# Attention and two expert layers on one core: heads of a pair on the two halves of the array, v as the stationary operand, tile loops written out

## The reference

```python
# attention: B=2, H=8, S=576, D=64
scores = scale * q @ k.T                      # scale = 1/8
kth = the 32nd largest score of each row
scores = where(scores >= kth, scores, -1e9)
attn = exp(scores - rowmax); attn /= attn.sum(-1) + 1e-9
x = attn @ v                                  # -> x: (1152, 512), token by (head, d)
# first layer: 1152 tokens, 512 -> 1536 -> 512
x = ((x @ w_a) * (x @ w_b)) @ w_out
# second layer: 4 experts, 512 -> 1024 -> 512
p = domain_probs / (domain_probs.sum(-1) + 1e-9)
out = sum over e of p[:, e] * (relu(x @ w1[e]) @ w2[e])
```

## Time and profile before

| | |
|---|---|
| median of 3 runs | 934.91 us (929.73, 935.0, 934.91) |
| the profiled execution | 931.27 us, span 929.5 us, so 1.8 us lie outside the span |
| PE busy (matmul) | 906.7 us, 98% of the span |
| DVE, ACT, POOL busy | 466.2, 356.3 and 386.4 us |
| mean granted PE clock | 0.969 of full speed |

### The profile page before, as it was taken

One profiled execution on the slowest core, in us unless ns is written; L12 is line 12 of the kernel. 1 busy time (PEld: TensorE's weight loads), 2 busy tenths in 40 slices (PEclk: granted clock), 3 DMA queues, 4 the chain that ended last, 5 costly groups with the idle time before them and its releaser, 6 DMA issues.

```text
span 929.5 us, 14737 instructions
## 1 busy us (share of the span) xinstructions
PE 906.7 (98%) x5012; PEld 803.7 (86%) x5012; DVE 466.2 (50%) x908; ACT 356.3 (38%) x748; POOL 386.4 (42%) x229
## 2 busy tenths in 40 slices
PE   6799999999999999999999999999999999999998
PEld 3567888888888888899999999889989988988997
DVE  4897899998888988962322222112112212221211
ACT  4465665655566656664332311023103301220110
POOL 2798877777666677672122130043003400070000
PEclk9575999999999999999999999999999999999999
DMA  7651000100000003313345020022000400000000
GB/s 200 134 137 41 16 24 23 30 26 24 24 24 26 24 23 115 115 39 104 102 148 216 1 90 2 0 89 92 0 0 8 173 0 0 0 0 23 11 34 34
DMA packets 63245, 50.40 MB, mean 54 GB/s; under 512 B 31840, under 2 KB 54368, under 8 KB 63200
## 3 DMA queue, kind: packets, MB, share of 16 engines
q1 hardware_dynamic: 58976, 43.55, 15.8%
q10 hardware_dynamic: 4224, 6.29, 2.1%
HBM read 40.39 MB, written 9.44 MB: 54 GB/s over the span
## 4 chain that ended last, share of the span: by engine, by line
PE 95%; SPq 2%; ACT 1%; DMA 1%; DVE 1%; issue 0%; ACTq 0%
PE ps L589 22%; PE ps L602 21%; PE ps L473 16%; PE ps L447 11%; PE ps L567 8%; PE ps L409 7%; PE ps L425 4%; PE ps L432 2%; PE ps L456 1%; SPq L265 1%; PE ps L406 1%; DMA v_sb<-v_in 1%; SPq L250 1%; PE ps L465 0%; SPq L256 0%
## 5 line engine op out<-in xcount | busy, mean ns | idle before, releaser
L985 POOL TENSOR_TENSOR w_lo<-w_raw,w_hi 128x2048 fp32r<-128x2048 f32 x16 | 74.1, 4654 | 307.8 <-ACT w_hi L695 307.8
L833 DVE MAX8 m<-work 128x8 f32<-128x576 f32 x216 | 152.3, 746 | 0.0
L770 ACT ACTIVATE h_hi<-ps 128x384 fp32r<-128x384 f32 x96 | 47.2, 492 | 272.5 <-PE ps L589 272.4
L944 POOL TENSOR_SCALAR p_sb<-s_sb,m 128x576 f32<-128x576 f32 x72 | 124.1, 1724 | 43.2 <-DVE m L833 43.2
L589 PE MATMUL ps<-x_hi,w_hi 128*128 128x384 f32 x384 | 128.5, 335 | 0.6 <-DVEq L906 0.6
L915 DVE SCALAR_TENSOR_TENSOR h_lo<-ps,h_hi 128x384 fp32r<-128x384 f32 x96 | 53.4, 557 | 150.1 <-ACT h_hi L770 150.0
L589 PE MATMUL ps<-x_lo,w_hi 128*128 128x384 f32 x384 | 128.4, 334 | 0.0
L589 PE MATMUL ps<-x_hi,w_lo 128*128 128x384 f32 x384 | 128.3, 334 | 0.0
L447 PEld LDWEIGHTS ps<-v_sb,pT 128*128 128x128 f32 (+3 forms) x800 | 101.0, 191 | 25.3 <-issue 15.3
L447 PE MATMUL ps<-v_sb,pT 128*128 128x65 f32 (+3 forms) x800 | 113.0, 282 | 2.1 <-ACT pT L651 2.1
L602 PE MATMUL ps<-w_lo,h_hi 128*128 128x512 f32 x288 | 113.5, 394 | 0.0
(11 more groups left out here) (87 smaller groups left out, 1589.5 us busy)
## 6 DMA issues: line engine op xcount, KB each, us to landing
w_raw<-moe_w_in SPq DMA_DIRECT2D x16, 1024.0 KB, 5.0
h<-hT SPq DMA_DIRECT2D x36, 192.0 KB, 2.1
h_raw<-h SPq DMA_DIRECT2D x9, 768.0 KB, 6.3
w_raw<-moe_w_a_in ACTq DMA_DIRECT2D x4, 768.0 KB, 6.3
w_raw<-moe_w_b_in ACTq DMA_DIRECT2D x4, 768.0 KB, 4.7
wo_raw<-moe_w_out_in SPq DMA_DIRECT2D x3, 1024.0 KB, 6.0
q_raw<-q_in SPq DMA_DIRECT2D x72, 32.0 KB, 2.2
v_sb<-v_in SPq DMA_DIRECT2D x18, 128.0 KB, 5.6
```

The source lines that it names most:

```text
L833: nc.vector.max(m8[:, par, i, 8 * r:8 * r + 8], work[:, i, :]).then_inc(ve_top, 1)
L944: nc.gpsimd.tensor_scalar(p_sb[:, ring, 0:S], s_sb[:, ring, :], m8[:, pr % 2, head, TOP_K - 1:TOP_K], None, ALU.is_ge).then_inc(po_m, 1)
L985: nc.gpsimd.tensor_tensor(lo[:, s, :], raw[s][:], hi[:, s, :].bitcast(F32), ALU.subtract).then_inc(done, 1)
```

## The change

Line numbers in the text are those of the kernel before, unless it says "after".

1. **Scores.** Both heads of a pair are done in one go, through four PSUM banks, head 0 and head 1 in turn, so that successive matmuls use rows 0 to 63 and rows 64 to 127 of the array. The four banks are shared with the transposes of p.
2. **Weighted sums.** v (128 keys by 64) is the stationary operand, the transposed p the moving one; the two heads write partitions 0 to 63 and 64 to 127 in turn. The result is x transposed, so the transpose of x falls away. The column of ones falls away too: the exponential of ACT gives the row sums (`accum_out`).
3. **Mask before exponential.** POOL adds -1e30 to the scores outside the 32 largest (`is_lt`, then `mult`, then an add), and ACT takes the exponential of that in place; before, the exponential came first and POOL multiplied it with the mask.
4. **Scaling.** The reciprocals are spread over the partitions by eight small matmuls with the identity (`inv_transpose`), copied by ACT (`inv_b`) and multiplied by POOL into x (`xu`); ACT makes the high part, POOL the low part.
5. **Order.** In a step of PE the h transpose stands ahead of both `up` products (before: between them), all transposes of p between them, and the weighted sums at the end. q of a whole tile is loaded and transposed at once; the first q is loaded by ACT's queue. On ACT both scores are copied together at the step's start.
6. **Loops.** All 44 steps are written out.

```diff
-            def scores(t, rep, pr, head):
...
-                pe.wait_ge(ac_s, n8)
-                rows = slice(head * D, (head + 1) * D)
-                for half in range(2):
...
-                        mm = nc.tensor.matmul(ps[:, half, 0:HALF], qT[rows, pr % 2, :], kT[rows, batch_of(rep), pr, cols],
-                                              start=True, stop=True)
+            def scores(n):
...
+                if n > LAG_PV:
+                    pe.wait_ge(ac_pT, 2 * (n - LAG_PV))
+                if n:
+                    pe.wait_ge(ac_s, 2 * n)
...
+                for half in range(2):
+                    cols = slice(half * HALF, (half + 1) * HALF)
+                    for tok, b in toks:
+                        for head in range(2):
+                            rows = slice(head * D, (head + 1) * D)
+                            mm = nc.tensor.matmul(ps[tok, 2 * head + half, 0:HALF], qT[rows, t % 2, pr, tok],
+                                                  kT[rows, b, pr, cols], start=True, stop=True)
+            def p_transpose(n):
+                for head in range(2):
+                    pe.wait_ge(ac_e, 2 * n + head + 1)
+                    pe.wait_ge(ac_s, 2 * min(n + LAG_PV, NP - 1) + head + 1)
...
+                for tok, b in toks:
+                    for c in range(KC):
+                        for head in range(2):
+                            mm = nc.tensor.matmul(ps_x[head * D:(head + 1) * D, pr * P + tok.start:pr * P + tok.stop],
+                                                  v_sb[b][:, c, 2 * pr + head, :], pT[:, head, c, tok],
+                                                  start=c == 0, stop=c == KC - 1)
+            def inv_transpose(t):
+                pe.wait_ge(ve_den, 2 * t + 2)
+                pe.wait_ge(ac_t, T_USE["inv", t])
+                for h in range(H):
+                    mm = nc.tensor.matmul(ps_t[h % 2 * D:(h % 2 + 1) * D, h // 2 * P:(h // 2 + 1) * P],
+                                          x_inv[:, h:h + 1].to_broadcast([P, D]), ident[:], start=True, stop=True)
...
+                m = unit_of(n)
+                if stored_of(n) is not None:
+                    h_transpose(stored_of(n))
+                if m is not None:
...
+                    up(wa_hi, wa_lo, ps_a, m, pe_a)
+                if pair_of(n) is not None:
+                    p_transpose(pair_of(n))
+                if m is not None:
...
+                    up(wb_hi, wb_lo, ps_b, m, pe_b)
+                if next_q(n) is not None:
+                    q_transpose(next_q(n))
+                if scaled_tile(n) is not None:
+                    inv_transpose(scaled_tile(n))
+                if pair_of(n) is not None:
+                    weighted_sum(pair_of(n))
...
+            def exponentials(n, head):
+                t, h = n // PR, 2 * (n % PR) + head
+                slot = p_sb[:, (2 * n + head) % 4, 0:S]
+                act.wait_ge(po_p, 2 * n + head + 1)
...
+                copy(slot, slot, ACT.Exp, scale=SCALE, bias=nmax[:, n % 2, head:head + 1],
+                     accum_out=x_sum[:, t % 2, h:h + 1]).then_inc(ac_e, 1)
...
+                if 0 <= n - 1 < NP:
+                    exponentials(n - 1, 1)
...
+                if n < len(SLICES):
+                    slice_hi(n)
...
+            def mask(n, head):
+                j, slot = 2 * n + head, (2 * n + head) % 4
...
+                nc.gpsimd.tensor_scalar(p_sb[:, slot, 0:S], s_sb[:, slot, :], m8[:, n % 2, head, TOP_K - 1:TOP_K], WORST,
+                                        ALU.is_lt, ALU.mult).then_inc(po_m, 1)
+                pool.wait_ge(po_m, j + 1)
+                nc.gpsimd.tensor_tensor(p_sb[:, slot, 0:S], p_sb[:, slot, 0:S], s_sb[:, slot, :], ALU.add).then_inc(po_p, 1)
+
+            for n in range(LAST + 1):
+                t, m = scaled_tile(n), unit_of(n)
+                if 0 <= n - 1 < NP:
+                    mask(n - 1, 0)
+                if t is not None:
+                    pool.wait_ge(ac_xu, t + 1)
+                    pool.wait_ge(ac_t, T_USE["inv", t] + 1)
+                    nc.gpsimd.tensor_tensor(xu[:], xu[:], inv_b[:], ALU.mult).then_inc(po_x, 1)
+                if 0 <= n - 1 < NP:
+                    mask(n - 1, 1)
...
+                if m is not None:
+                    pool.wait_ge(ac_a, m + 1)
+                    pool.wait_ge(ac_b, m + 1)
...
+                    nc.gpsimd.tensor_tensor(h_sb[:], a_sb[:], b_sb[:], ALU.mult).then_inc(po_h, 1)
+                if n < len(SLICES):
...
+                    pool.wait_ge(ac_w, n + 1)
```

More of the change, by code:

```diff
@@ L162, in build @@
         ld_v = [sem("ld_v0"), sem("ld_v1")]
-        ld_q = [sem(f"ld_q{i}") for i in range(PR)]
+        ld_q = sem("ld_q")
         ld_w = [sem(f"ld_w{i}") for i in range(RAW)]
@@ L401, in scores @@
                 for half in range(2):
                     cols = slice(half * HALF, (half + 1) * HALF)
-                    if rep == SPLIT:
-                        for b in range(2):
-                            tok = slice(b * (P // 2), (b + 1) * (P // 2))
-                            mm = nc.tensor.matmul(ps[tok, half, 0:HALF], qT[rows, pr % 2, tok], kT[rows, b, pr, cols],
-                                                  start=True, stop=True)
-                    else:
-                        mm = nc.tensor.matmul(ps[:, half, 0:HALF], qT[rows, pr % 2, :], kT[rows, batch_of(rep), pr, cols],
-                                              start=True, stop=True)
@@ L470, in up @@
+            def up(w_hi, w_lo, bank, m, done):
+                t, pr = divmod(m, PR)
                 cols = slice(pr * FS, (pr + 1) * FS)
@@ L654, in o_out @@
-            def o_out(t, pr, head):
-                act.wait_ge(pe_o, t * (2 * PR) + (2 * pr + head + 1))
-                if pr == 0 and head == 0:
-                    act.wait_ge(po_x, t)
-                copy(xu[:, 2 * pr + head, :], ps_o[:, 0:D + 1], ACT.Copy).then_inc(ac_o, 1)
-            def back(t, p, lag):
-                b = -(-(lag - p) // PR) if lag > p else 0
-                return t - b, p - lag + b * PR
+                act.wait_ge(ac_k, (PR + 1) * b + 2)
+                act.sem_inc(ac_t, 1)
@@ new lines, in scores_out, with negated_top @@
+            def scores_out(n):
+                for head in range(2):
+                    act.wait_ge(pe_s, n + 1)
+                    if n >= 2:
+                        act.wait_ge(po_p, 2 * (n - 2) + head + 1)
+                    copy(s_sb[:, (2 * n + head) % 4, :].rearrange("p (a c) -> p a c", a=2), ps_sc[head], ACT.Copy).then_inc(ac_s, 1)
+            def negated_top(n):
+                act.wait_ge(ve_top, TOPN * n + 2)
+                if n >= 2:
+                    act.wait_ge(ac_e, 2 * n - 2)
+                copy(nmax[:, n % 2, :], m8[:, n % 2, :, 0], ACT.Copy, scale=-SCALE).then_inc(ac_n, 1)
@@ L768, in relu @@
+            h_out(NP - 1)
             def relu(e, g, m):
```

734 lines of the change are left out of this document (305 added, 429 removed).

## The result

The changed kernel takes **972.38 us** (median of 4 runs, 971.71 to 972.64) against 932.32 (4 runs, 929.66 to 935.0) on the same chip: ratio 1.0429, 95% interval 1.0387 to 1.0471. It is slower by 4.3%, where some 2% were forecast. The profiled execution took 972.64 us, its span is 970.9.

| us | before | forecast | after |
|---|---|---|---|
| start to unit 8 | 102.71 | 114.2 | 122.30 |
| unit 8 to unit 35 | 298.59 | 283.6 | 302.55 |
| unit 35 to w_out | 50.07 | 64.0 | 65.11 |
| w_out to the end of the span | 478.1 | 478 | 480.9 |
| clock, apart | | +8 | in the rows above |

What follows compares the result with a forecast made beforehand. PE was taken to bound the kernel at 10.82 us a unit, with DVE close behind at 9.64. 931.3 + 11.5 (start) - 15.0 (middle) + 13.9 (end) = 941.7, plus 8 for the clock: 950, range 928 to 978.

Steps and rivals of the forecast that it cites:

- The overlap: PE's scores and weighted sums: both heads run at once on array halves, 1.17 and 1.20 us for both heads.
- The serial chain at the start: Steps 0 to 7: masks, exponential, high part and low part never overlap, 12.8 us a step; unit 8 comes 11.5 later.
- The tail: Unit 35 to the w_out product: PE waits for h in the last steps, 64.0 us, 13.9 more than 50.1.
- Chain (b): Third step of a tile: POOL waits for the spread reciprocals before scaling, so the next unit starts 12.1 us after, not 9.64.
- chain (c): Behind chain (b), once a tile: PE idles 5.7 us before the h transposes; the following unit starts 10.2 us later.
- three things that I had named as signs of being wrong: High parts ready before the masks, DVE waiting for nothing in the middle, or the clock falling for long stretches.
- The mask costs POOL more with two operations: Rival on POOL's mask: between 1.71 and 1.71 + 1.41 us, about 1000 us at the upper end; chance 0.05.
- I take 1.25 per fall: Clock falls at PE's gaps: 7 falls and one before step 39, 10 us, less up to 2 hidden by slack.
- I take 0.4 from POOL to another engine: Hand-overs between engines: 0.4 us from POOL to another engine, 0.1 elsewhere.
- nothing changes: After the pipeline, from 451.37 us on: the remaining 478 us stay.
- The clock holds: Rival: PE's clock does not fall in the gaps; 942 us, or 933 with short hand-overs; chance 0.27.
- DVE sets the pace throughout: Rival in the middle: chains (b) and (c) hide, units take 9.74 us, 921 in all; chance 0.10.

Runs made afterwards that it cites:

- slice_early: The changed kernel with ACT making the slice's high part (units 0 to 7) ahead of the exponentials instead of behind both: ratio 1.028 to the kernel before.
- mask_one_op: The changed kernel with POOL's mask only comparing, its multiplication by -1e30 left out (part of the computation is missing): ratio 1.019 to the kernel before.
- gap_filled_ready: The changed kernel with two unneeded products of the previous tile's x put into PE's gap before the h transposes: ratio 1.024 to the kernel before.
- mask_and_gap: The changed kernel without the mask's multiplication and with PE's gap before the h transposes filled by a ready product: 934.0 us, ratio 1.003.
- the reordered kernels: The changed kernel with four orders altered (918.6 us), then also sums ahead of the a product once a tile (915.7), then also 32 bytes of padding (912.2).

## Why the prediction was wrong

**Right:** the direction, and the three places. *The overlap* of both halves (1.17 and 1.20 forecast from start to start, 1.17 and 1.24 measured). *The serial chain at the start*, shown by slice_early. *The tail*, 64.0 forecast and 65.1 measured, with 1.71 us of waiting per step. *Chain (b)*, POOL waiting for the reciprocals, and *chain (c)*, PE idle for 5.7 us once a tile (5.82 measured), are both there, and the fall of the clock behind it. That chain (b) came out at 12.38 against 12.1 is luck: with the mask at the 1.72 us that it assumed, the unit is 10.73 (mask_one_op). And none of the three things that I had named as signs of being wrong happened, because they asked after the chains and not after the mask's price.

**Wrong, first step: "The mask costs POOL more with two operations ... Nothing in the trace shows it, and I take 1.71".** It had a bound of 1.71 + 1.41, and I took the lower end because no row showed more. It measured 2.21. That is only a third of the way to the upper end, but it stands twice in each step of a serial chain: 1.2 us for each of the units 3 to 7, 9.3 at the start, 15.9 in the middle and 1.1 at the end. My chains were short here too: with 2.21 put into them the whole would have risen by 12 us, to 962 (7 at the start, 3.5 in the middle, 1.5 at the end), not by the 26 that the distances give. mask_one_op is the kernel that I had costed: ratio 1.019, which on the profiled 931.3 us is 949, against 950 forecast, and its distances are 113.0, 286.6 and 64.0 where I had 114.2, 283.6 plus most of the clock's 8, and 64.0. This one term is nearly the whole miss: 1.043 less 1.019 is 22 us (the profiled executions, on two chips, differ by 26), and so is 972 less 950.

**Wrong, second step: "I take 1.25 per fall".** A fall costs 2.0 to 2.5 us in the middle, and the filler gave 17 us in all against my 8 (gap_filled_ready). The term came from the "some 2.5 us" that the clock had taken to come back before, a time that none of the rows shown has. What counts here is how much PE work falls into the stretch at the lower level: 4.75 and 4.98 us were busy in the two stretches above. There were also more falls than my 7 and 1, two of them in the first four units. In mask_one_op, where falls were also there, some of them shorter, this was balanced by chains that I had made some 6 us too long (mask_and_gap, 278.0 against 283.6). One term of these is *"I take 0.4 from POOL to another engine"*: the hand-overs took 0.04 to the exponential (72.54 to 72.58) and 0.06 to PE (291.10 to 291.16). With 0.1 for it my own sum was 933 instead of 942. Errors of opposite sign lie behind the good agreement just named. One more term goes the other way: the scaling took 1.27 us and not 1.04.

**Wrong, third: "nothing changes" after the pipeline.** The instructions are the same and their buffers are not: 3.5 us, of which 0.7 came back in w_out.

**The rivals.** "The clock holds" did not happen. "DVE sets the pace throughout" was given 921 and 0.10: it needs POOL's factors early, and the reordered kernels, in which most units run at DVE's pace, come to 912 to 919.

**Not tried.** No run takes back the written-out loops (point 6 of the change) or the new handling of q, so what these are worth is not shown.

**Where the gain went.** Forcing the halves apart puts 2.6 us of PE time back into every unit, its waits included; by that the overlap is worth some 38 us where it stands and 60 in a good order. The gain was lost to waits that the same edit made: h transposes first in PE's step, the scaling between two masks, the slice behind both exponentials, and a mask 0.49 us dearer on the engine that all wait for. All but the last are order, not work.

## What to carry to other kernels

When a change takes work off the busiest engine, write down the chain that takes over, and in it each operation at its dearer bound: a surcharge of 0.5 us on a serial chain cost 2.4% here. In each engine's queue ask of every instruction behind a wait whether it needs that wait; four moved orders turned 4% slower into 1.4% faster. And a gap on PE can slow the work behind it: here filling it, even with useless matmuls of ready operands, paid 2.0 to 2.5 us a time.

## What the runs showed of the hardware

- On POOL a tensor_scalar over 128x576 f32 takes 1724 ns with one operation and 2213 with two.
- With one head behind the other, PE still overlaps the two halves whole in the scores (8 instructions, 1.25 us against 1.24 alternating and 2.52 with a wait between), and in part in the sums (20 instructions, 2.02 us against 1.31 and 2.62).
- A PE gap of 5.8 us in a stretch that was dense otherwise brought the granted clock to its lower level for 6.8 us; twice 2.1 us of matmuls inside it kept it at 1.00.
- Shifting buffers by 32 bytes changed 128x512 matmuls by 0.5 to 1.3% (394 to 399 ns at most), some 3.5 us in all.
- On POOL the multiplication of 128x512 by a whole tensor takes 1.27 us, where that by a broadcast factor took 1.04.
- Each exponential that also sums is followed by a read of its accumulator, 0.19 us on ACT.
